# Regrouping the probability-times-value products of an attention stage: bursts of two, two and one key blocks in place of one, one, one and two

## The reference

```python
scores = scale * np.matmul(q, k.transpose(0, 1, 3, 2))
thresh = np.max(scores, axis=-1, keepdims=True) - tau
scores = np.where(scores >= thresh, scores, -1000000000.0)
attn = np.exp(scores - np.max(scores, axis=-1, keepdims=True))
attn = attn / (np.sum(attn, axis=-1, keepdims=True) + 1e-09)
x = np.matmul(attn, v)            # then heads side by side: 2304 x 512
h = x @ w_in;   x = (h - np.tanh(h)) @ w_out
h = x @ w2_in;  x = (h / (1 + np.exp(-h))) @ w2_out
```

## Time and profile before

| | |
|---|---|
| median of 3 runs | 1100.23 us (1100.09 to 1100.81) |
| profiled execution | 1100.23 us, its span 1098.4 us |
| PE busy | 1076.1 us (98%) |
| DVE, ACT, POOL busy | 559.1, 402.8, 265.5 us |
| granted clock of TensorE | 1.00 on average |
| pv matmuls (L683) | 640 instructions, first at 34.6 us, last at 305.3 us |

### The profile page before, as it was taken

The page is one execution under the profiler, slowest core; times in us unless marked ns, Lnnn a source line. Parts: engine busy times, 40 slices in busy tenths (PEclk is TensorE's granted clock), DMA queues, the critical chain, the costliest instruction groups (busy, mean ns, idle before and its releaser), DMA issues.

```text
span 1098.4 us, 15693 instructions
## 1 busy us (share of the span) xinstructions
PE 1076.1 (98%) x5808; PEld 870.5 (79%) x5808; DVE 559.1 (51%) x1342; ACT 402.8 (37%) x830; POOL 265.5 (24%) x240
## 2 busy tenths in 40 slices
PE   5999999999999999999999999999999999999998
PEld 4667677676678888888888889888888888888898
DVE  7999999999767543343343344622322322222222
ACT  5889898888732211121121121422211211111111
POOL 3767676776254200000000000444000000000000
PEclk9999999999999999999999999999999999999999
DMA  6334242431142100000000000232100000010010
GB/s 153 81 74 111 57 111 66 102 89 36 58 147 96 58 1 1 1 0 0 0 0 0 0 1 1 89 111 70 39 1 1 28 10 0 0 38 0 0 39 20
DMA packets 15195, 46.38 MB, mean 42 GB/s; under 512 B 2080, under 2 KB 2592, under 8 KB 15136
## 3 DMA queue, kind: packets, MB, share of 16 engines
q1 hardware_dynamic: 15136, 45.62, 14.8%
HBM read 40.89 MB, written 4.72 MB: 42 GB/s over the span
## 4 chain that ended last, share of the span: by engine, by line
PE 95%; DVE 1%; ACT 1%; POOL 0%; issue 0%; DVEq 0%; ACTq 0%
PE hid L761 36%; PE acc L777 35%; PE scores L718 9%; PE pv L683 8%; PE tps L740 6%; DVE x_lo L605 0%; ACT w_parts L450 0%; ACT x_hi L459 0%; DVE probs L584 0%; DVE probs L552 0%; ACT pT L407 0%; POOL q_parts L361 0%; DVE w_parts L635 0%; DVE stats L568 0%; ACT pR L409 0%
## 5 line engine op out<-in xcount | busy, mean ns | idle before, releaser
L761 PE MATMUL hid<-x_hi,w_parts 128*128 128x512 f32 (+1 forms) x1280 | 384.9, 368 | 3.2 <-DVE x_lo L605 2.1
L777 PE MATMUL acc<-g_hi,w_parts 128*128 128x512 f32 (+1 forms) x1280 | 384.1, 368 | 0.0
L761 PEld LDWEIGHTS hid<-x_hi,w_parts 128*128 128x128 f32 x1280 | 234.2, 189 | 44.6 <-DVE x_lo L605 2.2
L777 PEld LDWEIGHTS acc<-g_hi,w_parts 128*128 128x128 f32 x1280 | 234.1, 189 | 39.9
L761 PE MATMUL hid<-x_lo,w_parts 128*128 128x512 f32 (+1 forms) x640 | 235.4, 368 | 0.0
L777 PE MATMUL acc<-g_lo,w_parts 128*128 128x512 f32 (+1 forms) x640 | 235.4, 368 | 0.0
L619 DVE CAST g_hi<-h_act 128x512 fp32r<-128x512 f32 (+1 forms) x160 | 71.2, 445 | 270.0 <-ACT h_act L474 267.3
L374 POOL TENSOR_TENSOR w_parts<-w_raw,w_parts 128x1024 fp32r<-128x1024 f32 x30 | 73.6, 2457 | 400.0 <-ACT w_parts L450 399.9
L614 DVE TENSOR_TENSOR h_act<-hid,h_act 128x512 f32<-128x512 f32 (+1 forms) x80 | 51.0, 638 | 200.8 <-ACT h_act L471 200.8
L471 ACT ACTIVATE h_act<-hid 128x512 f32<-128x512 f32 (+1 forms) x80 | 44.4, 555 | 293.3 <-PE hid L761 293.3
L474 ACT ACTIVATE h_act<-hid 128x512 f32<-128x512 f32 (+1 forms) x80 | 44.4, 555 | 290.0 <-PE hid L761 290.0
(11 more groups left out here) (46 smaller groups left out, 765.9 us busy)
## 6 DMA issues: line engine op xcount, KB each, us to landing
w_raw<-w_in SPq DMA_DIRECT2D x32, 512.0 KB, 3.4
k_raw<-k_in SPq DMA_DIRECT2D x30, 288.0 KB, 4.8
q_raw<-q_in SPq DMA_DIRECT2D x30, 288.0 KB, 5.9
v_all<-v_in SPq DMA_DIRECT2D x16, 320.0 KB, 3.1
out<-xT SPq DMA_DIRECT2D x4, 1024.0 KB, 4.2
k_raw<-k_in SPq DMA_DIRECT2D x4, 144.0 KB, 3.0
q_raw<-q_in SPq DMA_DIRECT2D x4, 144.0 KB, 2.9
out<-xT SPq DMA_DIRECT2D x1, 512.0 KB, 2.9
```

The source lines that it names most:

```text
L761: last = pe.matmul(hid[f % HBANKS][:, 0:w], a, b[:, kc, 0:w], start=(kc == 0 and i == 0), stop=(kc == KC - 1 and i == 2))
L777: last = pe.matmul(acc[n][:, 0:w], a, b[f % GRING][:, 0:w], start=(f == 0 and i == 0), stop=(f == FT - 1 and i == 2))
```

## The change

Half 0 of a pair: blocks (0), (1), (2), (3, 4) at lags 8, 9, 10, 11 behind L_T become (0, 1), (2, 3), (4) at lags 8, 10, 11. Half 1: the same four groups at lags 12 to 15 become the same three at lags 13, 15, 16. The copy of half 0 stays at lag 12, the copy of half 1 goes from lag 16 to lag 17, and with it the loops' end TAIL from 57 to 58.

```diff
-L_PV = {L_T + 8: (0, 0, 1), L_T + 9: (0, 1, 2), L_T + 10: (0, 2, 3), L_T + 11: (0, 3, 5),
-        L_T + 12: (1, 0, 1), L_T + 13: (1, 1, 2), L_T + 14: (1, 2, 3), L_T + 15: (1, 3, 5)}
-L_OUT = {L_T + 12: 0, L_T + 16: 1}
+L_PV = {L_T + 8: (0, 0, 2), L_T + 10: (0, 2, 4), L_T + 11: (0, 4, 5),
+        L_T + 13: (1, 0, 2), L_T + 15: (1, 2, 4), L_T + 16: (1, 4, 5)}
+L_OUT = {L_T + 12: 0, L_T + 17: 1}
```

## The result

| | before | after |
|---|---|---|
| median | 1100.23 us | 1106.87 us (five runs, 1106.68 to 1108.49) |
| ratio | | 1.0059, 95% interval 1.0048 to 1.0070 |
| profiled execution, its span | 1100.23, 1098.4 us | 1108.49, 1106.7 us |

The change made the kernel 6.6 us slower; 1106.1 was forecast, in a range of 1102.0 to 1108.5.

What follows compares the result with a forecast made beforehand. PE was taken to bound the kernel by about 1 us per pair. First pair -0.7, pairs 1 to 13 +5.6 and tail +1.0 gave +5.9 us on 1100.23: 1106.1 us, range 1102.0 to 1108.5.

Steps and rivals of the forecast that it cites:

- PE is the bound before: Attention steps of the kernel before: PE takes 17.56 us a pair, DVE alone 16.6, so PE bounds by about 1 us.
- 0.34 us for a burst: PE's fixed price for going into and out of a burst; six in place of eight save 0.68 us a pair.
- Wait for the bank: At place 3 PE waits 0.65 us for ACT's copy of half 1, queued behind the rounding of the queries.
- Second wait: At place 1 PE's scores wait 0.44 us for DVE to free the score tile of place 8.
- This is set by PE: ACT's start on place 2's transposes, 1.27 us after the scores start; removing the 0.44 us copy ahead brings it no earlier.
- The first rival: Score tiles do not bind, so no wait for them at place 1: 17.55 us per pair, 1100.5 us; chance 0.10.
- The sum: Whole kernel: 0.43 us slower for each of 13 pairs, 5.6 us, with -0.7 and +1.0 makes +5.9 us.
- the first pair: Start of the attention steps: no half stands before this pair, so it keeps its 0.7 us gain.
- the tail: After the last scores: ACT's copy of half 1 and the last transpose come later, delaying the first hidden product 1.0 us.
- The third wait: DVE's row-sum close waits for ACT's exponential; margin 0.25 us, if gone by 0.3 us 1110 us; chance 0.05.
- The values' later load, banks and POOL at nothing: SP's load of values 2 us later, the transposes' PSUM banks and POOL's scaling: all costed at nothing.

Runs made afterwards that it cites:

- four_bursts: Against the kernel before: each half in two bursts of 2 and 3 blocks (lags 8, 10 and 13, 15), copies at lags 12 and 16; 1090.65 us.
- half0_only: Against the kernel before: only half 0 regrouped (2, 2, 1 blocks at lags 8, 10, 11), half 1 and its copy unchanged; 1095.54 us.
- half1_only: Against the kernel before: only half 1 regrouped and shifted (lags 13, 15, 16, copy at 17), half 0 unchanged; 1111.27 us.
- copy_early: Against the changed kernel: ACT's copy of half 1 moved one step earlier, in front of the rounding of the queries; 1099.39 us.
- shift_only: Against the kernel before: nothing regrouped, half 1 and its copy one step later (lags 13 to 16, copy at 17); 1105.79 us.
- less_dve_after: Against the changed kernel: DVE's addition of 1e-9 to the row sums left out; 1107.67 us.
- half_mask_after: Against the changed kernel: DVE masks only the first 288 of the 576 keys; 1104.51 us.

## Why the prediction was right, point by point

- **PE is the bound before, by about 1 us a pair.** Right for which engine, high for how much: halving the masking left 17.56; taking PE time out by regrouping without the shift gave 17.22 and then 16.91, where PE still ran without a wait (16.90 by the prediction's own sum). `four_bursts` puts the floor behind it at 16.92, so the room was 0.64 us, not 1. Nine tiles of 1.84 us are 16.6; the timeline of DVE there has one distance of 2.10 us, at the long scores, for which it still waits 0.18, and one of 1.90.
- **0.34 us for a burst.** Right: `half0_only` gave exactly that per pair, and `half1_only` against the change gave it once more. The Trainium skill's page "TensorEngine Tiling (Array Packing)", Key Properties, says that changing the tiling mode drains the engine. It gives no price, and no run here shows whether the drain is what makes up the 0.34 us.
- **Wait for the bank, 0.65 us.** Right in place and cause, measured 0.68. `copy_early`, `shift_only` and the two kernels with more work on ACT show it from three sides.
- **Second wait, 0.44 us, for the score tiles.** Measured 0.46, so the total came out right; but its weight was mis-stated, which matters for the rival and not for the total. "This is set by PE", said the prediction of ACT's start at place 2. That holds only because the second wait holds PE back. ACT's own chain from place 0 on is 0.1 us shorter than the way through DVE and the score tiles, so with DVE faster the pair is only 0.13 us shorter (18.05 to 17.92), not 0.44. The two are nearly parallel paths of one loop. The first rival, which dropped the second wait and put 17.55, was therefore wrong also on its own premise: without that wait it is 17.92. With `copy_early` ACT's path to the copy is 0.57 us shorter, and so is the pair (18.05 to 17.48).
- **The sum.** Per pair 0.43 was forecast and 0.49 measured, which is 13 x 0.06 = 0.8 us and the whole miss; 0.04 of the 0.06 stand in the rows above at the bank, where PE goes on at +4.09 and not at +4.05. The other two terms, -0.7 for the first pair and +1.0 for the tail, came out right together, +0.3 against +0.28 measured, but not one by one; that their errors cancel is luck. The first pair is only 0.11 us shorter. Its first period holds the bursts of half 0 alone, one fewer than before and not two, and DVE, which runs there without a gap from its tile at 27.84 to its tile at 40.74, makes PE wait 0.29 us for a score tile (transposes at 36.44, scores at 37.20, 0.76 where PE takes 0.47; DVE had begun its next tile at 37.06). In the tail, from `split_x` to the roundings of the weights it is indeed 1.10 us longer, but `split_x` itself starts 0.73 us sooner behind the last long scores (294.29 to 298.78, against 288.04 to 293.26), because one burst of two blocks now stands between the transposes that ACT copies ahead of it, in place of three of one block, and ACT no longer waits 0.58 us for the last of them. The prediction had nothing for that. Measured: start +0.09, first period -0.11, 13 periods together +6.3, last period -0.07, long scores to hidden product 12.40 against 12.03, +0.37. Sum 6.6 us.
- **The third wait** (DVE for the exponential) did not come in the changed kernel; with half masking, where DVE comes sooner, it did, 13 times, 0.2 us on average. That fits a margin as thin as was thought.
- **The values' later load, banks and POOL at nothing.** Right: in the list of waits of the kernel after nothing waits for `v_all` by name, `copy_early` rules the values out at place 3, and no transpose of PE waits.

## What to carry to other kernels

When one buffer is handed over between two engines, look at what stands ahead of the releasing instruction in its engine's queue, from that engine's last idle moment on, not only in the same step. A regrouping that saves time on the bound engine can be right and still lose through where its last piece ends; here one lag (14 and 15 in place of 15 and 16) is the difference between 1106.9 and 1091.6 us, half of it by the order on ACT and half by where the blocks stand on PE. And two waits in one loop are not two terms of a sum: take one away and see, before counting on it, which path is next.

## What the runs showed of the hardware that was not expected

**The clock at the change of layers.** The 1.65 us that the profiled execution lost beyond the change is in one place. The windows of the kernel after:

```profile
706.00:708.00 2.00, 0.97 (x3) 0.79 (x4) 2.00 (x3) 0.66 (x1) 0.43 (x1) 0.89 0.55 162
708.00:710.00 2.00, 2.00 (x6) 1.60 (x5) 0.85 (x3) 1.68 (x2) 1.53 (x1) 0.50 0.65 242
710.00:712.00 2.00, 2.00 (x8) 1.55 (x8) 0.51 (x2) 1.17 (x2) 0.84 (x1) 0.75 0.08 8
```

The granted clock falls to 0.50, that is 1.2 GHz, and is back at 2.4 GHz before 712 us. Just before, PE stood idle for 0.31 and 1.74 us, waiting for DVE's `x_lo` at the start of the second layer:

```profile
704.36 0.47 PE L761 MATMUL hid<-x_hi,w_parts 128*128 128x512 f32 x1 [0.31 <-DVE x_lo L605]
...
707.03 0.50 PE L761 MATMUL hid<-x_hi,w_parts 128*128 128x512 f32 x1 [1.74 <-DVE x_lo L605]
```

The profiled execution of the kernel before has waits of 0.32 and 1.74 us at the same spot and kept its clock at 1.00 there. Of the other profiled executions, those of `copy_early`, `less_dve_after`, `half_mask_after` and `four_bursts` show the same drop behind the same two waits, and the seven others show the waits without it. So the same gaps sometimes cost about 1.6 us and sometimes nothing; 5 of 15 executions of the kernel before, run beside the first experiments, took 1101.6 to 1101.95 us where the other ten took 1100.0 to 1100.24. The 13 bank waits of 0.68 us in the changed kernel left the clock at 1.00 in its profile. What tips it was not tried.

**A small operation that is free.** DVE's addition of 1e-9 (0.15 us) lies entirely within the 0.85 us from the start of the maximum to the statistics that depend on it. Taking it out left the tiles 1.84 us apart and the period at 18.05.
